# Expert routing between attention and two expert layers: 16-bit paired comparisons on VectorE, 128-column weights, earlier row transposes

## The reference, cut to what matters

```python
def _attn_ref(q, k, v, centroids):          # 2 batches, 8 heads, 768 rows, 64 columns, 16 clusters
    ...                                     # nearest centroid of each query and key; attention inside a cluster
def _moe_ref(x, w_gate, w1, w2):            # x 1536 x 512, 8 experts, 512 -> 1024 -> 512
    logits = x @ w_gate
    order = np.argsort(-logits.flatten())
    assigned = -np.ones(N); counts = np.zeros(E); cap = N // E      # cap = 192
    for idx in order:
        tok, e = idx // E, idx % E
        if assigned[tok] >= 0 or counts[e] >= cap:
            continue
        assigned[tok] = e
        counts[e] += 1
    for e in range(E):
        mask = assigned == e
        out[mask] = np.maximum(x[mask] @ w1[e], 0.0) @ w2[e]
def _moe2_ref(x, domain_probs, w1, w2):     # 4 dense experts, weighted by the row's probabilities
    for e in range(4):
        out += p[:, e:e + 1] * (np.maximum(x @ w1[e], 0.0) @ w2[e])
```

## Time and profile before

| | us |
|---|---|
| median of 3 runs | 1056.09 (1056.0 to 1059.53) |
| the profiled execution | 1053.91 |
| its span, first to last instruction | 1052.1 |
| TensorE busy in the span | 1011.7 (96%) |
| VectorE, ScalarE, GpSimd busy | 617.7, 485.3, 438.8 |
| routing and first expert layer | about 301 to 548 |

### The profile page before, as it was taken

The page is one execution under the profiler, slowest core; times in us unless marked ns, Lnnn a source line. Parts: engine busy times, 40 slices in busy tenths (PEclk is TensorE's granted clock), DMA queues, the critical chain, the costliest instruction groups (busy, mean ns, idle before and its releaser), DMA issues.

```text
span 1052.1 us, 17855 instructions
## 1 busy us (share of the span) xinstructions
PE 1011.7 (96%) x6392; PEld 927.4 (88%) x6392; DVE 617.7 (59%) x1306; ACT 485.3 (46%) x953; POOL 438.8 (42%) x359
## 2 busy tenths in 40 slices
PE   5999999999977999999999999999999999999996
PEld 4889999999966999999998999988999988899995
DVE  5788888888866555552405555444578544555542
ACT  4788888888810333336332332332353232233320
POOL 5043332324001111111466865655647855665542
PEclk9999999999975999999999999999999999999999
DMA  4233323332155657569932122212212412221201
GB/s 116 69 80 80 88 76 91 80 80 57 30 122 126 155 171 178 175 171 275 182 95 81 41 81 80 62 59 81 73 49 80 141 43 79 80 60 61 81 1 60
DMA packets 87744, 99.60 MB, mean 95 GB/s; under 512 B 18560, under 2 KB 57472, under 8 KB 87680
## 3 DMA queue, kind: packets, MB, share of 16 engines
q1 hardware_dynamic: 84976, 92.40, 32.2%
q0 software_dynamic: 2704, 6.33, 2.1%
HBM read 79.81 MB, written 6.32 MB: 82 GB/s over the span
## 4 chain that ended last, share of the span: by engine, by line
PE 91%; DVE 4%; ACT 2%; DMA 1%; POOL 1%; issue 1%; SPq 0%; DVEq 0%; ACTq 0%; POOLq 0%
PE ps_y L1452 9%; PE ps_y L1453 9%; PE ps_y L1451 9%; PE ps_h L1478 8%; PE ps_y L1493 8%; PE ps_h L1453 6%; PE ps_h L1451 6%; PE ps_h L1452 6%; PE ps_t L1356 6%; PE ps_s L1343 4%; PE ps_o L1370 3%; PE ps_o L1371 3%; PE ps_s L1344 3%; PE ps_m L1317 2%; PE ps_m L1390 2%; PE ps_y L1555 2%
## 5 line engine op out<-in xcount | busy, mean ns | idle before, releaser
L577 POOL TENSOR_TENSOR w_lo<-w_sum,w_hi 128x1792 fp32r<-128x1792 f32 x32 | 129.8, 4080 | 62.3 <-ACT w_hi L795 62.3
L1453 PE MATMUL ps_y<-b_lo,h_hi 128*128 128x512 f32 x384 | 149.7, 390 | 0.0
L1452 PE MATMUL ps_y<-b_hi,h_lo 128*128 128x512 f32 x384 | 149.7, 390 | 0.0
L1451 PE MATMUL ps_y<-b_hi,h_hi 128*128 128x512 f32 x384 | 149.4, 389 | 0.0
L1270 DVE SCALAR_TENSOR_TENSOR Y<-ps_y,mix_n,Y 128x512 f32<-128x512 f32 x84 | 63.0, 750 | 134.9 <-PE ps_y L1453 134.9
L1451 PE MATMUL ps_h<-x_hi,w_hi 128*128 128x384 f32 x384 | 128.6, 335 | 0.0
L1453 PE MATMUL ps_h<-x_lo,w_hi 128*128 128x384 f32 x384 | 128.5, 335 | 0.0
L1452 PE MATMUL ps_h<-x_hi,w_lo 128*128 128x384 f32 x384 | 128.4, 334 | 0.0
L583 POOL TENSOR_TENSOR b_lo<-b_raw,b_hi 128x2048 fp32r<-128x2048 f32 x16 | 74.0, 4627 | 115.9 <-ACT b_hi L802 115.9
L1001 DVE TENSOR_TENSOR p_lo<-ps_t,p_hi 128x384 fp32r<-128x384 f32 x192 | 99.9, 548 | 29.0 <-ACT p_hi L725 27.5
L992 DVE TENSOR_REDUCE neg_max<-ps_s 128x1 f32<-128x768 f32 x96 | 91.2, 950 | 17.0 <-PE ps_s L1344 17.0
(11 more groups left out here) (203 smaller groups left out, 2290.3 us busy)
## 6 DMA issues: line engine op xcount, KB each, us to landing
w_sum<-in_moe_w_dram SPq DMA_DIRECT2D x64, 256.0 KB, 3.2
b_raw<-in_moe_w_dram SPq DMA_DIRECT2D x16, 1024.0 KB, 5.2
raw_a<-in_moe_w_dram SPq DMA_DIRECT2D x8, 1024.0 KB, 9.6
raw_b<-in_moe_w_dram SPq DMA_DIRECT2D x8, 1024.0 KB, 13.3
odd_a<-in_moe_w_dram SPq DMA_DIRECT2D x8, 1024.0 KB, 9.2
odd_b<-in_moe_w_dram SPq DMA_DIRECT2D x8, 1024.0 KB, 15.3
khhT<-kqT SPq DMA_DIRECT2D x32, 192.0 KB, 2.9
raw_k<-in_k_dram SPq DMA_DIRECT2D x16, 192.0 KB, 2.4
```

Of the source, the lines that this page charges most:

```text
L577: g.tensor_tensor(w_lo[t][:], w_sum[t][:, 1:8], w_hi[t][:].bitcast(F32), ALU.subtract).then_inc(wlo_done[t], 1)
L1451: t_.matmul(dst, w_hi, x_hi, start=first, stop=False)
L1452: t_.matmul(dst, w_lo, x_hi, start=False, stop=False)
L1453: return t_.matmul(dst, w_hi, x_lo, start=False, stop=last)
```

## The change

It consists of six things.

1. `steps`, `level`, `cur`, `slot` and the new `dig_0` are held in bf16 instead of f32 (or int32), and values that are spread over levels or slots are stored twice side by side, so that both operands of the comparison are walked in pairs of neighbouring elements.
2. `slot_hot` is made by VectorE for all eight experts (`slots_hot`), behind `take_slots` and ahead of the next phase's work. ScalarE's `slot_far` and `slot_hot` instructions are gone.
3. All 12 counting matmuls and all 24 of `slot_tokens` have weights of 128 columns; the superfluous columns are stale or belong to the neighbour, and their outputs aren't read.
4. `token_ids(n - 1)` and `slot_tokens(n - 1)` come ahead of the first digit in every phase, no longer in the second digit.
5. The rows of expert 0 are transposed ahead of the third count of phase 1. The first unit comes ahead of its fourth count.
6. The tables of fills are new. Units per phase from phase 1 on: 13, 80, 64, 64, 64, 64 (before: 19, 59, 64, 64, 64, 64); then 9, 7, 9 instead of 12, 17, 16.

```diff
-    F_FIRST = (0,) * 7 + (2, 5, 2, 6, 4)
-    F_SECOND = (14, 2, 0, 2, 5, 2, 6, 2, 6, 2, 6, 4)
-    F_PHASE = (16, 2, 0, 2, 5, 2, 6, 2, 6, 2, 8, 2)
-    F_TOKENS = [0, 0, 8] + [11] * (E - 4)
+    F_FIRST = (0,) * 6 + (3, 1, 3, 1, 5, 0)
+    F_SECOND = (14, 2, 10, 2, 9, 2, 9, 2, 9, 2, 11, 0)
+    F_PHASE = (12, 2, 7, 2, 6, 2, 6, 2, 6, 2, 9, 0)
+    F_TOKENS = [0, 0, 8] + [8] * (E - 4)
-    WARM = [(30, 0, 18, 0, 12, 0, 12, 0, 12, 0, 16, 0), (14, 0, 18, 0, 12, 0, 12, 0, 0, 0, 0, 0)]
+    WARM = [(30, 0, 11, 0, 8, 0, 8, 0, 8, 0, 15, 0), (20, 0, 11, 0, 0, 0, 0, 0, 0, 0, 0, 0)]
+    W_TOKENS = [0, 16] + [0] * (E - 3)
...
-            def slot_far_tiles(n, tiles):
...
-            def slot_hot_tiles(n):
...
             for n in range(E - 2):
-                if n > 0:
-                    between_tiles(n, range(H_SPLIT[n - 1], 2 * KF))
-                    slot_hot_tiles(n)
                 results_and_rows(n)
-                for j in range(H_SPLIT[n]):
+                for j in range(2 * KF):
                     hidden_1(n, j)
...
+            def slots_hot(n):
+
+                hot = [P, NT, CAP // 2, 2]
+                dve.wait_ge(slot_ready, n + 1)
+                at_least(dve, ids_full, n)
+                v_.tensor_tensor(slot_hot[:, 0:NT * CAP].rearrange("p (t c two) -> p t c two", t=NT, two=2),
+                                 spread(steps[:].rearrange("p (c two) -> p c two", two=2), 1, hot),
+                                 spread(slot[:, n % 2], 2, hot), ALU.is_equal).then_inc(hot_ready, 1)
...
                 link(v_.tensor_reduce(pick[:], m2[:], AX.X, ALU.max))
+                add(v_.tensor_copy(dig_0[:], spread(dig_i[:, 0, :], 2, [P, NT, 2])))
                 add(v_.tensor_tensor(cand[:], m2[:], spread(pick[:], 2, shape), ALU.is_equal))
 
-                if n == 1:
-                    token_ids(0)
+                if n > 0:
+                    token_ids(n - 1)
+                dve.wait_ge(r_step, r_count[0])
...
-                    ks = [P, NT, K]
-                    v_.tensor_tensor(reach[:, :, 0:K], spread(now, 2, ks), spread(level[:, i, 0:K], 1, ks),
+                    ks = [P, NT, K // 2, 2]
+                    v_.tensor_tensor(reach[:, :, 0:K].rearrange("p t (k two) -> p t k two", two=2),
+                                     spread(now, 2, ks),
+                                     spread(level[:, i, 0:K].rearrange("p (k two) -> p k two", two=2), 1, ks),
                                      ALU.is_ge).then_inc(reach_ready, 1)
...
-                    if i == 1 and n > 1:
-                        token_ids(n - 1)
...
                 take_slots(n)
-                dve.wait_ge(slot_ready, n + 1)
-                if n == 0:
-                    first_slots_hot()
+                slots_hot(n)
...
             take_slots(E - 1)
             token_ids(E - 2)
+            slots_hot(E - 1)
             token_ids(E - 1)
...
-                    if k == 0:
-                        gathered_rows(0)
...
-                        mm = t_.matmul(ps_tok[0:HS, 2 * s:2 * s + 2], slot_hot[:, t, s * HS:(s + 1) * HS],
+                        c = t * CAP + s * HS
+                        mm = t_.matmul(ps_tok[:, 2 * s:2 * s + 2], slot_hot[:, c:c + P],
...
-                    if n == 1 and i == 0:
-                        keep_running(20)
-                        slot_tokens(0)
-                    if n > 1 and i == 1:
+                    if n > 0 and i == 0:
                         products(F_TOKENS[n])
+                        keep_running(W_TOKENS[n])
                         slot_tokens(n - 1)
                     products(fill[2 * i])
                     keep_running(warm[2 * i])
+                    if n == 1 and i == 2:
+                        gathered_rows(0)
                     pe.wait_ge(reach_ready, ND * n + i + 1)
                     for t in range(NT):
-                        mm = t_.matmul(ps_cnt[0:K, 0:E], reach[:, t, 0:K], cand[:, t, :], start=(t == 0),
+                        mm = t_.matmul(ps_cnt[:, 0:E], reach[:, t, :], cand[:, t, :], start=(t == 0),
...
-            products(12)
+            products(9)
+            slot_tokens(E - 2)
+            products(7)
             slot_ranks(E - 1)
-            products(17)
-            slot_tokens(E - 2)
-            products(16)
+            products(9)
             slot_tokens(E - 1)
             products(2 * S_E * E - unit_at[0])
```

More of the change, by code:

```diff
@@ L185, in clustered_attention_two_moes @@
         dig = sb("dig", [P, ND - 1, NT], F32)
-        cur = sb("cur", [P, 2, NT], F32)
+        cur = sb("cur", [P, 2, NT, 2], BF16)
+        dig_0 = sb("dig_0", [P, NT, 2], BF16)
         same = sb("same", [P, NT], F32)
@@ L200, in clustered_attention_two_moes @@
         rank = sb("rank", [P, 2, NT], F32)
-        slot = sb("slot", [P, 2, NT], F32)
+        slot = sb("slot", [P, 2, NT, 2], BF16)
         pen = sb("pen", [P, NT], F32)
@@ L506, in search_constants @@
                                     ALU.add).then_inc(levels_in, 1)
+                g.memset(slot_hot[:, NT * CAP:], 0.0).then_inc(levels_in, 1)
             def split_head(h, b):
@@ L850, in y_out @@
                        ps_y[:, j, 0:2 * CAP].rearrange("p (c m) -> p c m", c=2)).then_inc(y_taken, 1)
-            act.wait_ge(levels_in, 4 * ND)
-            def between_tiles(n, tiles):
-                c = NT // len(tiles)
-                for k, j in enumerate(tiles):
-                    slot_far_tiles(n, range(c * k, c * k + c))
-                    hidden_1(n - 1, j)
             def results_and_rows(n):
@@ L1102, in take_slots @@
                                              op0=ALU.add, op1=ALU.mult))
-                v_.tensor_tensor(slot[:, n % 2, :], rank[:, 0, :], rank[:, 1, :], ALU.add).then_inc(slot_ready, 1)
-            def first_slots_hot():
-                hot = [P, NT, CAP]
-                v_.tensor_tensor(slot_hot[:], spread(steps[:], 1, hot), spread(slot[:, 0, :], 2, hot),
-                                 ALU.is_equal).then_inc(hot_ready, 1)
+                pair = [P, NT, 2]
+                v_.tensor_tensor(slot[:, n % 2], spread(rank[:, 0, :], 2, pair), spread(rank[:, 1, :], 2, pair),
+                                 ALU.add).then_inc(slot_ready, 1)
+            def slots_hot(n):
[5 more added lines that the diff above has]
+                                 spread(slot[:, n % 2], 2, hot), ALU.is_equal).then_inc(hot_ready, 1)
             def token_ids(n):
@@ L1156, in phase @@
                         dve.wait_ge(digit_full, ND * n + i + 1)
-                        link(v_.scalar_tensor_tensor(out=cur[:, (i + 1) % 2, :], in0=now, scalar=ps_rt[:, 0:1],
-                                                     in1=dig[:, i, :], op0=ALU.subtract, op1=ALU.add))
+                        link(v_.scalar_tensor_tensor(out=cur[:, (i + 1) % 2], in0=now, scalar=ps_rt[:, 0:1],
+                                                     in1=spread(dig[:, i, :], 2, [P, NT, 2]), op0=ALU.subtract,
+                                                     op1=ALU.add))
                     else:
@@ L1166, in phase @@
                                              op0=ALU.is_equal, op1=ALU.mult))
-                add(v_.tensor_scalar(over[:], now, found[:], None, ALU.is_gt))
+                add(v_.tensor_scalar(over[:], now[:, :, 0], found[:], None, ALU.is_gt))
                 link(v_.tensor_reduce(e_top[:], e_b[:], AX.X, ALU.max))
-                add(v_.tensor_scalar(same[:], now, found[:], None, ALU.is_equal))
+                add(v_.tensor_scalar(same[:], now[:, :, 0], found[:], None, ALU.is_equal))
                 link(v_.scalar_tensor_tensor(out=chosen_in[:, 0, :], in0=pick[:], scalar=e_top[:], in1=over[:],
```

31 lines of the change are left out of this document (8 added, 23 removed).

## The result

| | before | after |
|---|---|---|
| median | 1056.05 (1054.27 to 1059.53, 4 runs) | 1041.84 (1041.11 to 1043.03, 4 runs) |
| ratio to before | | 0.9863, 95% interval 0.9836 to 0.9889 |
| the profiled execution, its span | 1053.91, 1052.1 | 1042.0, 1040.2 |

The changed kernel is 1.4% faster, 1.8 us above the forecast of 1040.0 and inside its range. To see where the time came from, I cut the span at four places that each trace shows: the idle matmuls that open the routing (300.90 before, 301.23 after), the ranks of expert 1, the ranks of expert 6, and the first matmul of the second layer (548.28 and 536.41). What lies ahead of the first place and behind the last is nearly the same work.

The account below looks back on a forecast made before the run. The chain bounds the front, TensorE's list the middle, expert 6's gather the tail. 9.1 + 7.7 + 0.8 - 1.6 = 16.0 us off 1053.9 gives 1037.9; plus 2.2 to the median, 1040.0, range 1033 to 1050.

Parts of the forecast that it names:

- The comparisons: On VectorE, paired 16-bit operands halve the time per element: 0.96 and 0.56 us, and 1.36 for `slot_hot`.
- The front: Routing phases 0 and 1, bound by the VectorE-TensorE chain: 9.1 us gained, bounds 7 and 11.
- the landing of their rows: Phase 1, expert 0: rows land 6.16 us after their ids, as before, at 327.0.
- the price of turning the rows sooner: Phase 1: the third count, queued behind expert 0's transposes, stalls with TensorE's 1.8 us wait for rows.
- The middle: Phases 2 to 6, bound by TensorE's list: 7.7 us gained from cheaper counts and `slot_tokens`, without waits.
- the slower case: Phases 2 to 5: gathers land late behind a(n), 10 us instead of 3.1; 1066 us in all, chance 0.05.
- the lower bound of 0.29: Gain per changed count, if part of the 0.82 belongs to the one-column matmul with 64 rows, which stays.
- The tail: Last phases: 0.8 us gained in two `slot_tokens`, 1.6 lost to a longer stall for expert 6's rows.
- `slots_hot(7)` doesn't delay it: Tail: expert 6's ids wait for expert 7's ranks, 6.1 us after expert 6's; `slots_hot(7)` adds no delay.
- The rows of expert 6 in time: Tail rival: the gather is ready at 11.8, before 12.5; tail term +3.3, 1035.1 us, chance 0.26.
- No pairs: Rival: pairs aren't read as pairs; front gains 5.0, `slots_hot` waits cost 6.3; 1050.5 us, chance 0.12.

Follow-up runs that it names:

- the single reads: The changed kernel, but the comparisons and `slot_hot` read their value singly instead of from a pair of copies; 1056.62 us, ratio to before 0.9998.
- the kernel with the count first: The changed kernel, but expert 0's rows are turned behind phase 1's third count, with 0, 4, 3 units for 3, 3; 1043.40 us, ratio 0.9868.

## Why the prediction was right, and where it was off

*The number* owes something to luck. The forecast for the profiled execution was 1037.9, 16.0 less than before; it took 1042.0, 11.9 less. The median came within 1.8 of its forecast because I had added 2.2 for the distance between the profiled execution and the median of before, and in the changed kernel that distance is 0.2 the other way.

*The comparisons* are as forecast to a hundredth: 0.96, 0.56 and 1.36, and the single reads show the reason. The Trainium skill's rule on step 1 and repeated elements (Vector Engine (DVE) Microarchitecture Reference, section 5.1) holds by both kernels.

*The front*, 9.1 forecast, 8.0 measured. With the 0.33 of the start taken off, the ranks of expert 0 came at 315.9, as said, and their ids at 320.8. The term that was mis-sized is the landing of their rows: I carried over 6.16 us from ids to rows; it was 7.0. The gather's own landing went from 3.6 to 4.5 us. It is now issued closer behind the 2 MB of `raw_a` (317.43), with DMA share at 1.04 until 324; that fits, but no run tests it in the front. That gives transposes at 327.9 instead of 327.0, a wait of 2.47 instead of 1.8, and ranks of expert 1 at 338.1 instead of 337.0. I had called the stall there the price of turning the rows sooner; the kernel with the count first shows that the price is nothing within the scatter, and the units at half clock the longer path.

*The middle*, 7.7 forecast, 6.6 measured; ranks to ranks 134.55 instead of 133.4. No waits came, as forecast, and the gathers of experts 2 to 5 landed in 3.3 to 4.3 us, so the slower case didn't arise. The mis-sized term is the count: 0.38 forecast, 0.28 measured (3.57 less 3.29), just below the lower bound of 0.29, and for the reason given with that bound. I had put the whole difference between a 64-level and a 128-level digit down to the columns; 0.19 of it stands at the small matmul with 64 rows, which the change leaves. `slot_tokens` gave 0.45 instead of 0.4.

*The tail*, -0.8 forecast, -2.4 measured. The wait (3.87 for a forecast stall of 3.6) and its place (16.4 for 16.1) held. One step of it was wrong in its reasoning: "`slots_hot(7)` doesn't delay it". It does: the gather, 1.88 us on GpSimd, ends 0.87 later than it would without it. The number came out nearly right all the same: the ids were there at 6.93 instead of 7.1, and the path from ids to rows took 9.48 instead of the 9.02 carried over. The size that was off is the clock: I had it cost 1.0 to 1.5, about as before; the 64 records behind the wait took 12.1 instead of 10.96 before, so 1.1 more went there, and 0.15 in the transposes. It is not the longer wait that decides this: behind a wait as long, 3.91 us, in the kernel with the count first, they took 10.6, and its tail comes to -0.9. The -2.4 thus holds for this trace alone. The sum of the tail: 0.9 from two `slot_tokens`, -2.05 of idle, -1.1 and -0.15 of clock, -2.4.

*The rivals.* The rows of expert 6 in time: it didn't come here, but the ids moved 2.75 ahead bring it, and it is worth 3.8 of median, 3.5 by the ratios. What decides is the traffic: held back, the weights let the gather through (at least 3.8 us sooner). No pairs: refuted. Had it been so, the median would be 1056.6, 6.1 more than the 1050.5 I had put, and by the trace nearly all of that is the tail. With equal units the front gained 4.2 where I had 5.0, and the middle 2.9 where I had 2.7 (7.7 less five waits of 1.0); the tail lost 9.4 where I had 2.1, through rows that come 23.2 us after the ranks. Of these, GpSimd's hold-up explains about 2, and 4.5 stay open (above).

## What to carry to other kernels

Here a comparison with 16-bit operands took half the time per element only where each was walked in neighbouring elements; where a value is repeated, store it twice. In a dense stretch look at small matmuls by rows as well as by columns: full 128 x 128 weights were the cheapest form of each. Before a GpSimd gather on which TensorE will wait, write its ids as early as the list allows, and see that no long VectorE instruction begins between the ids and the gather; but one moved ahead of the ids costs more than it saves (the rows came 0.56 later). And compare two traces only by more than what traces with the same code differ by.

## What the runs showed of the hardware

- A gather on GpSimd that is issued while VectorE runs a long instruction with two operands waits for its end. Without one behind the ids a gather occupies GpSimd for 0.99 to 1.00 us and ends 1.29 after the ids; with one of 0.94, 1.36 and 2.56 us it takes up to 1.47, 1.88 and 3.08, and in each of the dense phases and in the tail of after it ends 0.86 to 0.88 us after the end of that instruction (in phase 1, 1.20). A gather that has begun isn't held: beside a comparison that began 0.06 us behind it, it took 0.93. The Trainium skill (SBUF — State Buffer, "Who interferes with whom") says that a VectorE instruction with two SBUF inputs contends with GpSimd instructions that read SBUF. A gather reads its ids there, and the traces agree with that rule. The section also infers that making descriptors isn't hindered; for a gather that has begun the traces agree with this too, but the start of a gather, and with it the landing, is put off.
- A bf16 matmul of one or eight columns between f32 ones costs TensorE 0.19 us more with 64 rows of weights than with 128 (25.87 to 25.29 in 64 units, three such matmuls). Twelve counting matmuls take 0.80 with 64 columns, 0.48 with 128. For the columns the Trainium skill (TensorE: Matmul & The Clock Gate, "Weight-path perf modes — Fast Weight Load (FWL) and DoubleRow") has a rule that agrees: faster loading of 16-bit weights where there are 128.
- Idle matmuls in a 3.9 us wait kept the granted clock at 1.00 behind it; 18 of them in a 2.4 us wait, where it was already 0.50, didn't bring it back sooner.
- Behind waits of 3.87 and 3.91 us with the same code around them the granted clock stayed at 0.50 for some 6 us in one trace and some 3 in the other.
